# An attention and two feed-forward networks on one core: the token-side combinations of a seven-product block multiplication placed between the operations of neighbouring blocks

## The chip, the cores and the metric

The kernel runs on one core of a Trainium2 chip. The metric is the device time of one execution in microseconds, the median of several runs. A core has TensorE (PE in the profile), VectorE (DVE), ScalarE (ACT), GpSimd (POOL) and SyncE (SP), which here only issues DMAs. Each engine runs its own instructions in order and waits on semaphores.

## What is computed

```
attention: 2 batches x 8 heads, 768 tokens, head size 64; queries and keys meet only
           where the signs of six projections (proj) agree; softmax with eps 1e-9
x   = the attention's output, 1536 tokens x 512
y   = (h - tanh(h)) @ w_out,     h = x @ w_in        (w_in 512 x 2048)
out = sum over 4 experts e of  p[:, e] * (relu(y @ w1[e]) @ w2[e])     (w1[e] 512 x 1024)
      p = domain_probs / (their sum over e + 1e-9)
```

All is float32. To keep float32 accuracy with TensorE's faster rounded format, each operand is split in a rounded part (hi) and the rest (lo), and each product is made of three: lo*hi + hi*lo + hi*hi.

## The kernel before

**Attention.** Sixteen heads go in eight pairs (`pair(it)`, it = 0 to 7), each pair in twelve tiles t of 128 queries. For a tile PE scores it, VectorE takes the row's extreme (`clamp`), ACT the exponential (`take_exp`), PE turns it, ACT rounds what was turned (`round_turned`, pT_hi), VectorE makes the rest (`rest_turned`, pT_lo), and PE multiplies with the values (`weigh`). POOL prepares the queries and keys of later heads, adds eps to the sums (`add_eps`), adds the halves of a result (`x_add`) and scales it into acc (`x_scale`). After the last pair the engines finish the last head: VectorE inverts its sums (`invert`), adds (`last_sum`) and scales it (`last_scale`) itself; the inverse goes by DMA through DRAM into inv_rows (`spread_inverse` on SP).

**The two networks.** The hidden units come in groups of 256: 8 groups in the first network, 16 in the second. A pass i takes two groups and has four blocks r = 0 to 3: r // 2 is the half b of the tokens (768 each), r % 2 the group. I1 = 4: blocks (0,0) to (3,3) belong to the first network, (4,0) = (I1,0) and later to the second. A block's upward product is made by seven products instead of eight (`product`, L1393, six matmuls each): both the weights and x^T are cut in quadrants, and sums of quadrants are multiplied. So there are seven combinations, slots 0 to 6, on the weight's side (`up_sums` on POOL, `up_round` on ACT, `up_rest` on POOL) and seven on the token side, made once for each call c: c = 0 and 1 for the two token halves in the first network, c = 2 and 3 in the second. Slots 0, 1, 2 are plain quadrants of acc, slots 3 to 6 sums: `x_sum` for slots 3, 4, 6 on VectorE (L989, xq_raw) and for slot 5 on POOL (L521); `x_round` on ACT (L728, xq_hi); `x_rest` for slots 0, 1, 3, 4 on VectorE (L1001, xq_lo) and for 2, 5, 6 on POOL (L530). The xq_raw of slots 3 to 6 lies in the place of xq_lo, so that the sum is overwritten by the rest.

**A block's order.** PE (`place_block`, L1433): product 0 (P0), P1, one tile of the previous block's downward product (D0), P3, D1, P4, the product with x slot 2 (P6,2), tiles D2 to D4, P5, the rest of the tiles, and the product with x slot 6 (P(2,6)). A tile of the first network is 384 wide and there are eight, in the second 512 and six. ACT copies what P0, P3 and P4 left (`take_c1`, `take_c5`, `take_c2`, L795, L800, L805), VectorE adds the other products (`first`, `second_part`, `third`, L1107, L1112, L1117) and takes the down tiles (`down`). Between them the nonlinearity: ACT's tanh (L782), VectorE's subtraction (`hidden_sub`, L1128), ACT's rounding (L810) and POOL's rest (`hidden_rest`, L616) in the first network; ACT's relu (L858) and VectorE's rest (`positive_rest`, L1197) in the second. P4 waits for c1, P(6,2) for c5, P5 for c2, and P(2,6) for `third`'s h22. `down_round` (L736) and `down_rest` (L1006) split the downward weights in blocks r = 0 and 1.

**Where the splits of x stand.** c = 0 lies in pairs 5 and 6 and one operation of pair 7, among the tiles. The others stand in one piece: c = 1 partly after (0,0), the rest after (0,1); c = 2 (`split_x(2)`) after (3,3) and c = 3 after (4,0), on all three engines:

```python
                for r in range(4):
                    stage1(I1 - 1, r)
                split_x(2)
                stage2(I1, 0, 0, 0, after1=True)
                split_x(3)
```

The upward weights of group 1 are loaded after pair 7, summed on POOL in block (0,0), rounded on ACT and finished on POOL there; block (0,1) is the first to use them. wu_raw holds one group at a time.

## Time and profile before

| | us |
|---|---|
| median of three runs | 1057.4 (1056.42 to 1058.4) |
| profiled execution | 1058.94 |
| its span, first to last instruction | 1056.9 |
| PE busy | 1005.9 (95%) |
| VectorE busy | 690.8 (65%) |
| ACT busy | 467.1 (44%) |
| POOL busy | 454.9 (43%) |

The span is one execution's; times in the rows count from its start. Attention runs to about 254 us, the first network to about 520 us, the second to the end. Matmuls are pipelined and their ends are modelled, so PE's busy time shows where it waits but not how close it is to its peak. The granted clock (PEclk) is a share of 2.4 GHz; it has two levels, 1.2 and 2.4 GHz, so that a share between is a mixture in time.

### The profile page before, as it was taken

The page shows a single profiled execution, that of the slowest core. Times are in us where ns is not written, and L with a number is a line of the kernel's source. Part 1 is how long each engine was busy: PE and PEld are TensorE (multiplying, and loading weights), DVE is VectorE, ACT ScalarE, POOL GpSimd, SP SyncE. Part 2 cuts the span into 40 slices and gives each one's busy share as a digit, 9 for nine tenths or more (in the row PEclk, how much of TensorE's full clock was granted, in tenths as well). Part 3 has the DMA queues.
Part 4 walks back from the last instruction along what each step waited for, and adds up shares of the span by engine and source line. Part 5 has one row for each costly group of instructions (what it writes and reads, how often), then busy time and mean ns, then how long its engine had stood idle before and what let it go on. Part 6 is the DMA issues. An engine that isn't in the chain of part 4 may idle for free.

```text
span 1056.9 us, 16509 instructions
## 1 busy us (share of the span) xinstructions
PE 1005.9 (95%) x5438; PEld 926.9 (88%) x5438; DVE 690.8 (65%) x1124; ACT 467.1 (44%) x850; POOL 454.9 (43%) x436
## 2 busy tenths in 40 slices
PE   7999999898789999999696999999999999999998
PEld 5999998787789999999686999989889889989987
DVE  6888888896765556465677555555655565565554
ACT  4788777877434434443542232323223232233321
POOL 3687778876456355462753221313223041221200
PEclk9999999999889999999998999999999999999999
DMA  4445454442100101010010010100101001010003
GB/s 128 136 130 147 128 133 133 127 122 65 40 1 21 60 20 40 19 53 27 20 41 20 21 40 20 55 24 20 60 20 40 20 21 58 20 59 13 27 1 119
DMA packets 48324, 59.50 MB, mean 56 GB/s; under 512 B 4928, under 2 KB 31648, under 8 KB 48288
## 3 DMA queue, kind: packets, MB, share of 16 engines
q1 hardware_dynamic: 48128, 58.68, 19.3%
q10 hardware_dynamic: 160, 0.39, 0.1%
q8 instruction: 16, 0.26, 0.1%
q14 instruction: 20, 0.16, 0.1%
HBM read 44.07 MB, written 3.19 MB: 45 GB/s over the span
## 4 chain that ended last, share of the span: by engine, by line
PE 58%; issue 6%; POOL 5%; DVE 3%; ACT 1%; POOLq 0%; DVEq 0%; ACTq 0%
PE ps L1398 27%; PE ps L1421 25%; PE ps L1429 6%; POOL wu_lo L550 2%; POOL g_lo L616 2%; DVE xq_raw L989 1%; DVE xq_lo L1001 1%; POOL wu_raw L540 0%; POOL wu_raw L536 0%; DVE acc L1142 0%; POOL wu_raw L543 0%; POOL wu_raw L538 0%; ACT g_hi L810 0%; ACT wd_hi L736 0%; ACT g_hi L858 0%
## 5 line engine op out<-in xcount | busy, mean ns | idle before, releaser
L1398 PE MATMUL ps<-xq_hi,wu_lo 128*128 128x384 f32 x672 | 230.8, 343 | 31.9 <-DVE xq_lo L1001 15.9
L1398 PE MATMUL ps<-xq_hi,wu_hi 128*128 128x384 f32 x672 | 229.0, 341 | 0.0
L1398 PE MATMUL ps<-xq_lo,wu_hi 128*128 128x384 f32 x672 | 228.9, 341 | 0.0
L550 POOL TENSOR_TENSOR wu_lo<-wu_raw,wu_hi 128x768 fp32r<-128x768 f32 (+1 forms) x48 | 106.7, 2238 | 252.9 <-ACT wu_hi L732 252.8
L1159 DVE SCALAR_TENSOR_TENSOR acc<-ps,p_norm,acc 128x512 f32<-128x512 f32 x180 | 134.9, 749 | 102.5 <-PE ps L1421 99.1
L1398 PEld LDWEIGHTS ps<-xq_hi,wu_lo 128*128 128x128 f32 x672 | 127.9, 190 | 41.7 <-issue 19.8
L1421 PE MATMUL ps<-wd_lo,g_hi 128*128 128x512 f32 x384 | 151.2, 394 | 0.0
L1421 PE MATMUL ps<-wd_hi,g_hi 128*128 128x512 f32 x384 | 151.1, 393 | 0.0
L1421 PE MATMUL ps<-wd_hi,g_lo 128*128 128x512 f32 x384 | 150.9, 393 | 0.0
L858 ACT ACTIVATE g_hi<-hb 128x384 fp32r<-128x384 f32 x96 | 50.3, 524 | 187.7 <-DVE hb L1117 121.8
L1398 PEld LDWEIGHTS ps<-xq_lo,wu_hi 128*128 128x128 f32 x672 | 128.2, 191 | 5.4
L1398 PEld LDWEIGHTS ps<-xq_hi,wu_hi 128*128 128x128 f32 x672 | 128.1, 191 | 0.0
L616 POOL TENSOR_TENSOR g_lo<-hb,g_hi 128x384 fp32r<-128x384 f32 x64 | 65.8, 1028 | 128.3 <-ACT g_hi L810 128.3
L687 ACT ACTIVATE prob<-prob,neg_max 128x768 f32<-128x768 f32 x96 | 90.2, 940 | 39.0 <-DVE prob L948 39.0
L955 DVE TENSOR_TENSOR pT_lo<-ps,pT_hi 128x512 fp32r<-128x512 f32 x144 | 94.5, 683 | 13.1 <-ACT pT_hi L694 12.4
L948 DVE TENSOR_SCALAR_CACHE_REDUCE prob<-ps 128x768 f32<-128x768 f32 x96 | 90.9, 948 | 5.2 <-PE ps L1315 5.2
L1326 PE MATMUL ps<-ident,prob 128*128 128x128 f32 x576 | 84.6, 278 | 9.0 <-DVE pT_lo L955 8.7
L1421 PEld LDWEIGHTS ps<-wd_hi,g_hi 128*128 128x128 f32 x384 | 72.2, 188 | 16.9
L1429 PE MATMUL ps<-g_hi,wd_lo 128*128 128x384 f32 x256 | 86.9, 340 | 0.0
L1429 PE MATMUL ps<-g_hi,wd_hi 128*128 128x384 f32 x256 | 86.8, 339 | 0.0
L1429 PE MATMUL ps<-g_lo,wd_hi 128*128 128x384 f32 x256 | 86.7, 339 | 0.0
L1142 DVE TENSOR_TENSOR acc<-ps,acc 128x384 f32<-128x384 f32 x112 | 61.4, 554 | 36.4 <-PE ps L1429 36.0
(118 smaller groups left out, 1814.9 us busy)
## 6 DMA issues: line engine op xcount, KB each, us to landing
wu_raw<-in_w SPq DMA_DIRECT2D x64, 128.0 KB, 2.4
wd_raw<-in_w SPq DMA_DIRECT2D x16, 512.0 KB, 3.4
q_raw<-in_qT SPq DMA_DIRECT2D x32, 192.0 KB, 3.2
k_raw<-in_kT SPq DMA_DIRECT2D x30, 192.0 KB, 3.3
wu_raw<-in_w_in SPq DMA_DIRECT2D x32, 128.0 KB, 2.3
wd_raw<-in_w_out SPq DMA_DIRECT2D x8, 512.0 KB, 3.5
v_raw<-in_vP SPq DMA_DIRECT2D x16, 192.0 KB, 2.8
inv_rows<-inv_dram SPq DMA_DIRECT2D x16, 192.0 KB, 3.2
```

What stands on the lines that cost most here:

```text
L550: rest = pool.tensor_tensor(wu[par][1][:, slots, :, :], wu_raw[:, slots, :, :], wu[par][0][:, slots, :, :].bitcast(F32), ALU.subtract)
L616: pool.tensor_tensor(g_lo[par][:, f, l * HALF:(l + 1) * HALF], hb[:, h, :], g_hi[par][:, f, l * HALF:(l + 1) * HALF].bitcast(F32), ALU.sub ...
L687: act.activation(prob[t % 3][:], prob[t % 3][:], ACT.Exp, bias=neg_max[:, t:t + 1], scale=-1.0, accum_out=total[:, t:t + 1]).then_inc(exp_ ...
L858: act.activation(to, u_ps[r % 2] if n == 3 else source, ACT.Relu).then_inc(g_hi_ready, 1)
L948: dve.tensor_scalar(prob[t % 3][:], score_ps[slot][:, 0:S], MASKED, None, ALU.min, ALU.min, accum_out=neg_max[:, t:t + 1]).then_inc(clampe ...
L955: dve.tensor_tensor(pT_lo_flat[:, cols], turn_ps[m % 3], pT_hi_flat[:, cols].bitcast(F32), ALU.subtract).then_inc(pT_lo_ready, 1)
L1142: dve.tensor_tensor(part_of, d_ps[k % 4][:, 0:HALF], part_of, ALU.add).then_inc(down_taken, 1)
L1159: dve.scalar_tensor_tensor(out=part_of, in0=source, scalar=scale, in1=part_of, op0=ALU.mult, op1=ALU.add).then_inc(down_taken, 1)
L1326: mm = pe.transpose(turn_ps[m % 3][:, at * P:(at + 1) * P], prob[t % 3][:, k * P:(k + 1) * P], ident[:])
L1398: mm = pe.matmul(to, w[:, wslot, k, :], x[:, xslot, k, :], start=start and k + m == 0, stop=k == 1 and m == 2, skip_group_check=not start)
L1421: mm = pe.matmul(to, x[:, f, rows], y[:, f, :], start=f + m == 0, stop=f == FC - 1 and m == 2)
L1429: mm = pe.matmul(to, x[:, f, rows], y[:, f, cols], start=f + m == 0, stop=f == FC - 1 and m == 2)
```

## The change

- The token-side combinations of c = 1, 2 and 3 all move to VectorE: slot 5's sum and the rests of slots 2, 5, 6 leave POOL. `stage1` and `stage2` get `begin` and `end`: in a block with `begin` VectorE makes the sums 3 and 4 and the rests of slots 0, 1, 3, 2, and in the next one, with `end`, the sums 6 and 5 and the rests of 4, 5, 6. They stand singly between the block's own operations, except in (0,0), where five of the six stand together after hidden_sub 2. The blocks are (0,0)/(0,1) for c = 1, (3,3)/(4,0) for c = 2, (4,1)/(4,2) for c = 3. ACT's roundings stand in the same blocks: 0 and 1 before the block's first tanh, 3 after the first rounding, 4 and 2 before the third part; 5 and 6 in the next block ahead of its weight roundings and of take_c2.
- PE waits for each slot's rest by itself, in the order in which the products use them.
- c = 0: the seven sums and rests on VectorE are cut in halves of 384 columns, one to a tile: t = 0 to 5 and 8 to 11 of pair 5, t = 5, 7, 9, 11 of pair 6. ACT's order of rounding becomes 0, 1, 3, 4, 2, 5, 6; POOL's rests of slots 2, 5 and 6 move by some tiles.
- Group 0's weights are rounded and finished two to three tiles earlier in pair 7. Group 1's are loaded in the middle of pair 7, summed at t = 9, rounded by ACT at t = 11 and finished on POOL before and after `add_eps(HEADS - 1, 1)` and `x_add`.
- (0,0): the last head's three `weigh` parts stand after P1, after P3 and before the down tiles instead of together; `move_last(1)` follows take_c2; `last_sum(1)` and both `last_scale` follow second_part.
- g_hi, g_lo and v_st change places in SBUF, so that group 1's weights can be written before the attention is over.

```diff
-        HI_ORDER = (0, 3, 2, 5, 1, 4, 6)
+        HI_ORDER = (0, 1, 3, 4, 2, 5, 6)
+        REST_ORDER = (0, 1, 3, 2, 4, 5, 6)
...
+                        if isinstance(it, int) and it == PAIRS - 1 and b == 0:
+                            sp.wait_ge(wu_lo_ready, 1)
+                            load_up(sp, w_in[:, G:2 * G])
...
-                            if t == 3:
-                                x_rest(0, 6)
-                            if t == 6:
-                                up_rest(0, 0, 0)
-                            if t == 7:
-                                up_rest(0, 0, 1)
+                            if t == 2:
+                                x_rest(6)
+                            if t in (3, 4):
+                                up_rest(0, 0, t - 3)
+                            if t == 9:
+                                up_sums(1)
...
                 pair(PAIRS - 1, last=True)
+                up_rest(1, 1, 0)
                 add_eps(HEADS - 1, 1)
                 x_add(PAIRS - 1, 0)
+                up_rest(1, 1, 1)
...
-                        if last and t == 4:
+                        if last and t == 2:
                             up_round(0, 0)
                         if last and t == 7:
                             down_round(0, 0)
+                        if last and t == TILES - 1:
+                            act.wait_ge(clamped, HEADS * QT)
+                            up_round(1, 1)
...
+                    if begin is not None and not start:
+                        x_round(begin, 0)
+                        x_round(begin, 1)
                     act.wait_ge(h11_ready, count_of(i, r) + 1)
                     take_tanh(i, r, 0, hb[:, 0, :])
...
+                    if begin is not None and not start:
+                        x_round(begin, 3)
+                    if end is not None:
+                        x_round(end, 5)
+                        x_round(end, 6)
...
+                        if isinstance(it, int) and it == PAIRS - 3 and t < 6:
+                            x_sum(0, (3, 4, 6)[t // 2], slice(t % 2, t % 2 + 1))
+                        if isinstance(it, int) and it == PAIRS - 3 and t >= 8:
+                            x_rest(0, DVE_REST[t // 2 - 4], slice(t % 2, t % 2 + 1))
...
                     down(0)
+                    if end is not None:
+                        x_sum(end, 6)
+                        x_rest(end, 4)
+                    if begin is not None and not start:
+                        x_sum(begin, 3)
                     hidden_sub(i, r, 0)
+                    if end is not None:
+                        x_sum(end, 5)
+                    if begin is not None and not start:
+                        x_rest(begin, 0)
                     down(1)
                     second_part()
                     down(2)
+                    if begin is not None and not start:
+                        x_sum(begin, 4)
+                    if start:
+                        last_sum(1)
+                        last_scale(0)
+                        last_scale(1)
                     hidden_sub(i, r, 1)
+                    if end is not None:
+                        x_rest(end, 5)
                     down(3, 4)
+                    if begin is not None and not start:
+                        x_rest(begin, 1)
...
+                stage1(0, 0, begin=1)
+                stage1(0, 1, end=1)
...
+                stage1(I1 - 1, 3, begin=2)
+                stage2(I1, 0, 0, 0, after1=True, end=2)
+                stage2(I1, 1, 0, 0, begin=3)
+                stage2(I1, 2, 0, 0, end=3)
+                stage2(I1, 3, 0, 0)
```

## Rows read from the trace of the kernel before

**Rows 1.** The page's 40 slices: granted clock of TensorE in tenths.
```profile
PEclk9999999999889999999998999999999999999999
```
**Rows 2.** Windows: length, then busy us (instructions) of PE, PEld, DVE, ACT, POOL, clock.
```profile
128.14:156.92 28.78, 28.75 (x189) 26.36 (x188) 24.68 (x50) 22.89 (x48) 22.41 (x28) 1.00 0.51 137
156.92:190.81 33.89, 31.50 (x191) 28.15 (x190) 29.97 (x54) 25.06 (x52) 27.40 (x30) 0.95 0.44 119
190.81:223.79 32.98, 29.61 (x192) 26.89 (x191) 28.05 (x52) 25.75 (x51) 26.88 (x30) 1.00 0.54 139
...
253.77:269.07 15.30, 10.40 (x59) 9.42 (x57) 8.96 (x12) 8.46 (x15) 10.54 (x10) 0.95 0.16 56
269.07:287.19 18.12, 18.12 (x90) 18.12 (x91) 11.62 (x19) 7.21 (x13) 5.58 (x5) 0.86 0.20 59
287.19:313.30 26.11, 18.68 (x92) 18.39 (x92) 20.12 (x22) 9.24 (x16) 13.73 (x9) 0.80 0.00 0
504.25:519.98 15.73, 15.73 (x91) 15.58 (x90) 8.64 (x16) 7.74 (x13) 10.79 (x11) 1.00 0.04 11
519.98:547.92 27.94, 18.72 (x91) 17.67 (x91) 21.83 (x22) 11.21 (x16) 18.27 (x11) 0.82 0.05 14
547.92:574.91 26.99, 18.02 (x80) 15.42 (x79) 23.57 (x24) 9.63 (x15) 15.03 (x8) 0.81 0.17 57
574.91:590.53 15.62, 15.62 (x79) 14.08 (x79) 8.13 (x13) 3.54 (x7) 0.00 (x0) 1.00 0.01 2
```
**Rows 3.** Waits of PE: who waited for whom, us in total, times, longest.
```profile
PE ps L1398 <- DVE xq_lo L1001: 15.9, 3, 8.2
...
PE ps L1398 <- ACT hb L800: 6.5, 1, 6.5
```
**Rows 4.** The chain of work in (0,2): start us, us, what.
```profile
288.10 2.62 DVE xq_raw L989
```
**Rows 5.** Timeline of DVE: start us, us, instruction, [idle before <-releaser].
```profile
254.54 1.29 DVE L955 TENSOR_TENSOR pT_lo<-ps,pT_hi 128x512 fp32r<-128x512 f32 x2
...
511.81 0.56 DVE L1112 TENSOR_TENSOR hb<-ps,hb 128x384 f32<-128x384 f32 x1 [1.55 <-PE ps L1398]
...
542.18 2.11 DVE L1197 SCALAR_TENSOR_TENSOR g_lo<-hb,g_hi 128x384 fp32r<-128x384 f32 x1
...
545.15 1.21 DVE L1006 TENSOR_TENSOR wd_lo<-wd_raw,wd_hi 128x1024 fp32r<-128x1024 f32 x1
...
548.94 0.96 DVE L989 TENSOR_TENSOR xq_raw<-acc 128x768 f32<-128x768 f32 x1
...
559.84 2.87 DVE L1001 TENSOR_TENSOR xq_lo<-xq_raw,xq_hi 128x768 fp32r<-128x768 f32 x2
...
568.83 0.75 DVE L1155 TENSOR_SCALAR acc<-ps,p_norm 128x512 f32<-128x512 f32 x1 [1.26 <-PE ps L1421]
```
**Rows 6.** Timeline of POOL, columns as before.
```profile
252.35 0.20 POOL L488 TENSOR_TENSOR total_eps<-total,eps 128x6 f32<-128x6 f32 x1 [3.32 <-ACT prob L687]
...
288.09 1.80 POOL L521 TENSOR_TENSOR xq_raw<-acc 128x768 f32<-128x768 f32 x1 [0.96 <-DVE acc L1083]
...
511.38 1.85 POOL L550 TENSOR_TENSOR wu_lo<-wu_raw,wu_hi 128x768 fp32r<-128x768 f32 x1
...
515.48 2.41 POOL L550 TENSOR_TENSOR wu_lo<-wu_raw,wu_hi 128x1024 fp32r<-128x1024 f32 x1
```
**Rows 7.** Timeline of ACT, columns as before.
```profile
253.40 0.48 ACT L708 ACTIVATE pv_other<-ps 64x384 f32<-64x384 f32 x1 [0.65 <-PE ps L1345]
...
507.00 1.71 ACT L732 ACTIVATE wu_hi<-wu_raw 128x1792 fp32r<-128x1792 f32 x1 [0.58 <-POOL wu_raw L543]
...
510.77 0.49 ACT L805 ACTIVATE hb<-ps 128x384 f32<-128x384 f32 x1 [0.44 <-PE ps L1398]
...
518.77 0.83 ACT L728 ACTIVATE xq_hi<-acc 128x768 fp32r<-128x768 f32 x1
...
539.52 1.04 ACT L736 ACTIVATE wd_hi<-wd_raw 128x1024 fp32r<-128x1024 f32 x1
```

More of the change, by code:

```diff
@@ L636, in stage1 @@
                         up_sums(2 * i + 2)
-                def split_x(c):
-                    x_sum(c)
-                    for slot in POOL_REST:
-                        x_rest(c, slot)
                 def stage2(i, r, more=True):
@@ L1191, in stage1 @@
                     hidden_sub(i, r, 2)
+                    if begin is not None and start:
+                        x_sum(begin, 3)
+                        x_rest(begin, 0)
+                        x_sum(begin, 4)
+                        x_rest(begin, 1)
+                    if begin is not None:
+                        x_rest(begin, 3)
+                    if end is not None:
+                        x_rest(end, 6)
                     down(6, 7)
+                    if begin is not None:
+                        x_rest(begin, 2)
                 def positive_rest(i, r, n, f, l):
@@ L1220, in stage2 @@
                     down(0)
+                    if end is not None:
+                        x_sum(end, 6)
+                        x_rest(end, 4)
+                    if begin is not None:
+                        x_sum(begin, 3)
                     positive_rest(i, r, 0, 0, 0)
+                    if end is not None:
+                        x_sum(end, 5)
+                    if begin is not None:
+                        x_rest(begin, 0)
                     down(1)
```

252 lines of the change are left out of this document (127 added, 125 removed).

## The prediction

> **What bounds the kernel now.** I read the page's clock slices first, then the windows by stage, then PE's waits, then the instructions of the bad stretches in order of time. The clock slices [rows 1] say where to look: TensorE holds its upper level, 2.4 GHz, except around 170 us, 265 to 315 us and 530 to 580 us. The windows [rows 2] give the price. A steady pair of heads takes 28.8 us with PE busy throughout, but the pair in which group 0 of the token side is combined takes 33.9 and the next 33.0: 9.3 us over. A steady block takes 15.7 us in the first network and 15.6 in the second. Against that block (0,1) takes 18.1, (0,2) 26.1, (I1,0) 27.9 and (I1,1) 27.0: 2.4 + 10.4 + 12.2 + 11.4 = 36.4 us over. (0,0) takes 15.3 for 42 products' matmuls and 12 of the attention, 54 at 15.7/90 = 0.174 us, 9.5 with the small turn: 5.8 us over. So the change's territory holds 51 us above steady running; the rest runs at PE's pace and gives nothing.
>
> PE's waits [rows 3] name VectorE's xq_lo for 15.9 us in three waits, the longest 8.2, and ACT's copy of z for 6.5, which was itself queued behind the split. The granted clock of those windows is 0.80 to 0.86 [rows 2]: after each long wait PE runs at 1.2 GHz for some microseconds, which is part of the excess.
>
> **What one combination costs.** Alone, an x operation on VectorE takes 0.96 us, next to POOL's operations of the split 2.6, and the chain shows why: it lasts 2.62 where POOL's own operation of 1.80 began 0.01 earlier [rows 4 to 6]. The two take turns: a VectorE operation with two SBUF inputs waits for POOL's running one and then needs 2.62 - 1.80 = 0.8 to 0.9. Beside POOL's shorter sums each takes 1.43 [rows 5]. (POOL's in turn waits.) So I cost an x operation at 0.96 plus what is left of POOL's operation: 0 to 2.4.
>
> **Part 1, attention (group 0 of x).** The same sums and rests stay on VectorE, but as 14 halves of about 0.5 us (the 384-wide operation, 0.56 to its end [rows 5]) where seven whole ones stood; ten fall in pair 5, four in pair 6. In the windows VectorE's busy time rises by 5.3 us for four operations and by 3.4 for three, 1.24 each, so meeting POOL costs 0.28 a time [rows 2]. Halves: 0.78 each, 7.8 and 3.1 us. Before, almost none of it was absorbed (5.1 and 4.2 us of growth for 5.3 and 3.4, the rest being ACT's roundings, which stay). VectorE idles 4.1 us in a steady pair; placed one to a tile, I let the halves use 3.0 of it in pair 5 and 1.5 in pair 6: 7.8 + 0.8 - 3.0 + 3.1 + 0.8 - 1.5 = 8.0, against 9.3. Gain 1. Bounds: nothing absorbed, 12.5 (3 worse); all 4.1 and 3.1 absorbed, 5.3 (4 better). The skill has a rule here, in the Trainium skill's Perfetto Trace Analysis, "Optimizing Scalar/DVE Operations": breaking up instructions can help where VectorE isn't saturated but makes others idle, each with an overhead of some 60 ns; by it alone the halves would sit at the better bound.
>
> **Part 2, the end of attention.** Group 1's weights are loaded, summed and rounded earlier: SP's four DMAs move ahead of the last inverse's, POOL's four sums to t = 9, up_round(1, 1) to the last tile of ACT, and up_rest(1, 1) on POOL to either side of add_eps. This removes the wait for wu_lo before (0,1) (part of (0,0)'s 5.8). But the 1.71 us rounding [rows 7] now stands on ACT ahead of the last two pT_hi. Worse, POOL's first rest, 1.85 [rows 6], waits for that rounding and stands ahead of add_eps (before: done at 252.55 [rows 6]), which VectorE's reciprocal waits for, and behind this are queued last_sum(0) and the two last pT_lo. ACT reaches the rounding at 253.9 [rows 7]: 253.9 + 1.7 + 1.85 + 0.2 = 257.7 for add_eps, then 0.2 + 0.6 + 1.29 [rows 5] gives pT_lo at 259.8, where it was 255.8. PE has two products until 256.0, then waits 3.8 us and probably drops to 1.2 GHz. From here on I set down end times, with my own allowance of 0.1 to 0.2 us for each step from engine to engine. The weigh parts now alternate with products and hide ACT's copies: part 0 261.1 at 1.2 GHz, P3 263.0, part 1 264.3, P4 265.7, P(6,2) 266.8, part 2 267.5, P5 268.6. VectorE: second_part 267.5, last_sum(1) after ACT's move_last 268.8, both last_scale 270.0 (I take inv_rows as landed), hidden_sub(1) 270.6, third 271.1. P(2,6) runs to 272.3, where (0,1) started at 269.07.
>
> **Part 3, c = 1, in (0,0) and (0,1).** In (0,0) ACT's roundings 0 and 1, 0.83 each [rows 7], stand ahead of tanh 2, so hidden_sub(2) ends at 274.1. Then six x operations run on VectorE in a lump, 5 x 1.0 and one that meets POOL's hidden_rest, 1.8: 280.9, and only behind them (0,1)'s hidden_sub and first(). ACT's roundings 3, 4, 2 and tanh 3 bring c1 to 280.6. PE does two products, two down tiles (D0 waits for hidden_rest until 276.0) and P3 by 279.1, then waits for P4 till 280.7. VectorE: first() 282.0, down(0) 282.5, sum 6 and rest 4 284.5, hidden_sub 285.1, sum 5 286.1. ACT: roundings 5 and 6 287.9, down_round, 1.04, 289.0, take_c2, 0.49 [rows 7], 289.4. P5 starts at 289.5 where D4 ended at 287.5; down_rest, 1.21, and x_rest(5) delay third() by another 1.2. (0,2) starts at 296.2 instead of 287.19 but then runs at 15.7 and not 26.1: (0,3) starts at 312 instead of 313.3. Gain 1. Bounds: if the end of attention hides its lump (3.8 less at part 2), 5; if 1.2 GHz lasts through (0,0), 3 worse.
>
> **Part 4, c = 2, in (I1-1,3) and (I1,0).** In (I1-1,3) ACT's two roundings delay c5 by 0.6 us, VectorE (8.6 us busy in a steady block [rows 2]) takes six more operations, and two of them meet POOL's wu_lo rests of 1.85 and 2.41 [rows 6]; up_rest of the next group also comes later, behind hidden_rest 1. (I1,0) starts at 521.5, not 519.98. There the 8.2 us wait is gone, since slots 0 to 3 are ready. New: VectorE enters 1.5 late, first() 525.6, down(0) 526.1, x_sum(6) behind hidden_rest 527.8, rest 4 behind one of POOL's sums 529.3; PE wanted P4 at 526.8 and waits 2.6. Then positive_rest(0) 530.4, x_sum(5) 531.9; ACT: roundings 5 and 6 533.6, up_round, 1.71, 535.3, down_round 536.3, take_c2 536.8; VectorE: second_part and down(2) 537.9, positive_rest(1), held by up_rest (2.11 beside the same work before [rows 5]), 540.1, x_rest(5) 541.0. PE was ready for P5 at 534.7 and waits 6.3, then runs a product at 1.2 GHz. The block ends at 548 as before (547.92). Gain 0; bounds: POOL met half as often, 4 better; the sums loaded later, 3 worse.
>
> **Part 5, c = 3, in (I1,1) and (I1,2).** POOL is idle in both but for sums. In (I1,1) VectorE's load is three adds of 0.56, four rests of 0.56, six tiles of 0.75, down_rest 1.21 [rows 5] and 6 x 0.96: 15.4 us in 15.6. It fits; third() comes 0.5 late. (I1,1) takes 16.1, not 27.0. In (I1,2), P4 waits 0.7 for slot 4 and P5 1.9 for slot 5 (x_sum(5), two roundings, c2, second_part, down(2), rest, x_rest(5) in a row), P(2,6) 0.9: 19.1 instead of 15.6. Gain 10.9 - 3.5 = 7.4. Bounds: 5 (every x operation meets a sum once more) to 11 (none of the new waits).
>
> The xsum, xlo and PE's new slot-by-slot waits cost nothing beside this: a wait already met is not seen in the rows. The memory moves change no row.
>
> **Sum.** 1 + 1 + 0 + 7.4 = 9.4 us. The profiled execution took 1058.9 with a span of 1056.9, 1.5 above the median 1057.4. 1058.9 - 9.4 - 1.5 = 1048.0.
>
> **Rivals.** (a) The single operations mostly find POOL idle and the queue behind them short. For it: POOL is busy for 10.8 of 15.7 us in a steady block with rests, but none in (I1,2) [rows 2]. Parts 1 to 5 then give 4 + 5 + 4 + 9 = 22: 1035. Chance 0.13. (b) The wait only changes its name: PE waits for take_c2 and h22 in all four blocks as long as it waited for xq_lo. For it: that is what part 4 gives. Against: at c = 3 POOL is out of the way. Then part 5 gives 2 and the others 0: about 1056. Chance 0.08. (c) Slower: VectorE becomes the bound through turn-taking with POOL. There are 33 x operations after attention; a steady block leaves VectorE 7.1 us [rows 2], six blocks 43. At 0.96 they need 32 and fit; at 2.6 each 86, 43 over, plus the 3.8 at the end of attention: 47 against the 42.2 now over in these blocks, so 1062. It decides from about 2.4 us a piece. Against: 2.6 occurs only where POOL runs the split itself, which goes away. Chance 0.06. The Trainium skill speaks against this move in the same section of Perfetto Trace Analysis: with VectorE saturated some work may go to GPSIMD, though sharing a port may spoil that. By it this rival decides; VectorE at 8.6 of 15.7 us isn't saturated. (d) My forecast: 0.73.
>
> **How the numbers follow.** The range reaches from near rival (a), 1037, to rival (b), 1056: it leaves out most of (a) and all of (c). A measurement of this kernel can tell about 0.2%, 2.1 us: faster means below 1055.3. (a), (d) and a quarter of (b) lie there, less a little of (d): 0.86; same 0.08, slower 0.06.
>
> **What would show it.** Right: PE's waits name xq_lo for under 6 us, and ACT's c2 copy or VectorE's h22 for more than before; one wait of 3 to 4 us before the first weigh after the last scores; (0,3) starting near 312 and the second network's second block near 548 with the third near 564; POOL's x operations three instead of twelve; pairs 5 and 6 together near 65.5 us. Wrong: no wait at the end of attention, (I1,0) in under 20 us, or x operations on VectorE with a mean above 2 us.

## The result, and the profile after

The changed kernel takes 1051.1 us in the median (1050.9 to 1051.8), beside 1057.3 (1056.4 to 1058.4) for the kernel before: ratio 0.994, 95% interval 0.9925 to 0.9959. The forecast was 1048.0 in a range of 1037 to 1056, with a chance of 0.86 for faster. The gain is 6.2 us and not 9.4. The profiled execution took 1051.0 with a span of 1049.2, against 1056.9 before.

First the clock slices, as in [rows 1]. One slice of 40 shows a share below 0.9, where three did. A 9 stands for anything from 0.9 up, so that shorter stretches at the lower level, such as those of the windows below, don't show here.

```profile
PEclk9999999999999999999989999999999999999999
```

Then the windows of the changed kernel that answer to [rows 2]: length in us, then busy us (instructions) of PE, PEld, DVE, ACT, POOL, the granted clock, the DMA share and GB/s. They are a steady pair, pair 5, pair 6, pair 7 up to the first product of (0,0), the blocks (0,0), (0,1), (0,2), and from 505.55 on (I1-1,3), (I1,0), (I1,1), (I1,2).

```profile
127.46:156.12 28.66, 28.62 (x189) 26.29 (x188) 24.67 (x49) 22.87 (x48) 22.41 (x28) 1.00 0.51 137
156.12:194.35 38.23, 33.83 (x205) 29.90 (x204) 34.91 (x59) 25.67 (x52) 27.81 (x31) 0.96 0.41 111
194.35:227.72 33.37, 28.71 (x175) 25.64 (x172) 28.09 (x54) 24.84 (x49) 24.46 (x28) 0.95 0.49 127
227.72:258.87 31.15, 28.73 (x189) 25.86 (x187) 27.12 (x51) 26.05 (x50) 23.39 (x24) 1.00 0.32 86
258.87:276.30 17.43, 11.73 (x58) 10.91 (x57) 7.51 (x13) 7.84 (x14) 8.16 (x6) 0.90 0.24 73
276.30:298.70 22.40, 18.26 (x91) 17.01 (x91) 18.79 (x26) 11.21 (x20) 4.30 (x4) 0.92 0.04 11
298.70:314.50 15.80, 15.80 (x93) 15.80 (x92) 9.25 (x18) 5.55 (x12) 5.50 (x6) 1.00 0.05 19
505.55:522.10 16.55, 16.17 (x92) 15.53 (x91) 12.09 (x17) 10.04 (x16) 10.51 (x9) 1.00 0.00 0
522.10:547.80 25.70, 19.75 (x90) 18.69 (x91) 19.54 (x26) 8.47 (x13) 11.41 (x8) 0.87 0.22 62
547.80:563.90 16.10, 16.06 (x79) 14.05 (x79) 11.68 (x18) 8.26 (x13) 2.88 (x4) 1.00 0.02 5
563.90:582.85 18.95, 16.34 (x80) 13.85 (x79) 14.41 (x21) 5.01 (x9) 0.00 (x0) 1.00 0.07 25
```

Reading it stage by stage against [rows 2], and against the place where each step was forecast to end:

| stage | before | forecast | after | gain |
|---|---|---|---|---|
| pair 5 to the first product of (0,0) | 96.9 | 95.5 | 102.8 | -5.9 |
| of it pairs 5 and 6 | 66.9 | 65.5 | 71.6 | -4.7 |
| first product of (0,0) to that of (0,3) | 59.4 | 58.2 | 55.6 | 3.8 |
| (I1-1,3) and (I1,0) | 43.7 | 43.7 | 42.3 | 1.4 |
| (I1,1) and (I1,2) | 42.6 | 35.2 | 35.1 | 7.5 |

Pair 5 also begins 0.8 us earlier in the profiled execution (156.12 for 156.92), so attention as a whole costs 5.1. The sum, -5.1 + 3.8 + 1.4 + 7.5 = 7.6, is the 7.7 us between the spans. The loss in attention, where a gain of 1 was forecast, is the large miss, and two other stages gave more than forecast. Each number is one profiled execution's; how far such stages repeat is said at the head of the experiments.

PE's waits, as in [rows 3] (who waited for whom, us in total, times, longest), name the same releasers with other sizes:

```profile
PE ps L1379 <- DVE pT_lo L968: 9.3, 8, 1.6
PE ps L1451 <- DVE xq_lo L1017: 8.6, 5, 4.1
PE ps L1451 <- DVE hb L1134: 2.2, 1, 2.2
...
PE ps L1451 <- ACT hb L799: 1.9, 1, 1.9
PE ps L1348 <- DVE inverse L1029: 1.8, 1, 1.8
...
PE ps L1398 <- DVE pT_lo L968: 1.7, 1, 1.7
PE ps L1451 <- POOL wu_lo L549: 1.4, 3, 0.5
...
PE ps L1451 <- ACT hb L794: 1.1, 2, 0.8
```

xq_lo fell from 15.9 to 8.6, ACT's copy c5, the forecast's "copy of z" (`take_c5`, hb, L794), from 6.5 to 1.1 in two, and the two waits at the end of attention (1.8 for the inverse, 1.7 for pT_lo before the first weigh) are new. The halves themselves can be seen in VectorE's timeline of pair 5 (start us, us, instruction, idle before it):

```profile
160.50 0.57 DVE L1003 TENSOR_TENSOR xq_raw<-acc 128x384 f32<-128x384 f32 x1
...
164.23 1.82 DVE L1003 TENSOR_TENSOR xq_raw<-acc 128x384 f32<-128x384 f32 x1
...
173.23 2.10 DVE L1003 TENSOR_TENSOR xq_raw<-acc,xq_raw 128x384 f32<-128x384 f32 x1
...
192.31 2.12 DVE L1017 TENSOR_TENSOR xq_lo<-acc,xq_hi 128x384 fp32r<-128x384 f32 x1
```

and beside them POOL's, same columns:

```profile
163.79 1.84 POOL L521 TENSOR_TENSOR xq_raw<-acc 128x768 f32<-128x768 f32 x1
...
173.08 1.83 POOL L475 TENSOR_TENSOR k_st<-k_raw,k_st 64x768 fp32r<-64x768 f32 x1
...
192.16 1.85 POOL L475 TENSOR_TENSOR k_st<-k_raw,k_st 64x768 fp32r<-64x768 f32 x1
```

Each long half starts 0.15 to 0.44 us behind an operation of POOL and ends 0.42 behind its end: 163.79 + 1.84 = 165.63 and 164.23 + 1.82 = 166.05; 174.91 and 175.33; 194.01 and 194.43. A half alone takes 0.55. The 14 halves take 16.4 us, 1.17 each; the forecast had 0.78 each, 10.9. The seven whole operations before took 9.3, which is 0.36 each above their own 0.96.

### The profile page after: what moved, and what is told of

Read it like the earlier page. It is cut to its first block, busy times and chain, and to the rows that moved or that the text cites. A ratio compares the mean times of both kernels' runs of the same rounds, so it can differ in the third digit from the quotient of the medians.

```text
span 1049.2 us, 16514 instructions
## 1 busy us (share of the span) xinstructions
PE 1006.5 (96%) x5438; PEld 924.4 (88%) x5438; DVE 687.4 (66%) x1143; ACT 466.9 (44%) x850; POOL 424.5 (40%) x424
## 3 DMA queue, kind: packets, MB, share of 16 engines
q1 hardware_dynamic: 48128, 58.68, 19.5%
## 4 chain that ended last, share of the span: by engine, by line
PE 74%; DVE 9%; issue 8%; POOL 6%; ACT 2%; DMA 1%; POOLq 0%; SPq 0%; ACTq 0%; DVEq 0%
PE ps L1451 27%; PE ps L1474 24%; PE ps L1482 6%; PE ps L1368 5%; PE ps L1398 5%; PE ps L1379 4%; PE ps L1342 2%; POOL wu_lo L549 2%; POOL g_lo L617 2%; DVE xq_lo L1017 2%; DVE xq_raw L1003 2%; DVE pT_lo L968 1%; DVE prob L961 1%; ACT xq_hi L719 1%; POOL wu_raw L539 0%
## 5 line engine op out<-in xcount | busy, mean ns | idle before, releaser
L1451 PE MATMUL ps<-xq_hi,wu_lo 128*128 128x384 f32 x672 | 229.5, 342 | 15.9 <-DVE xq_lo L1017 8.6
L1379 PEld LDWEIGHTS ps<-ident,prob 128*128 128x128 f32 x576 | 67.9, 141 | 20.0 <-DVE pT_lo L968 14.4
```

The source lines that it names most:

```text
L1379: mm = pe.transpose(turn_ps[m % 3][:, at * P:(at + 1) * P], prob[t % 3][:, k * P:(k + 1) * P], ident[:])
L1451: mm = pe.matmul(to, w[:, wslot, k, :], x[:, xslot, k, :], start=start and k + m == 0, stop=k == 1 and m == 2, skip_group_check=not start)
```

## The experiments

All times are medians of 4 to 10 executions, to be held against 1051.1 for the changed kernel. They were taken on three chips, on which the kernel before had medians of 1058.0 (the first four experiments), 1056.8 (one input, c2 ahead, group 3 as before, the parts together) and 1057.0 (the last four), so a difference of 1 us or less says nothing. The second number given is the length of a stage in the trace, one execution each. Behind attention, stages with the same code repeat within 1.1 us: from the first product of (0,0) to that of (0,3) five kernels that are alike there (the changed one, whole operations, one input, group 3 before, group 3 in a lump) took 55.6, 56.5, 56.5, 56.7 and 55.8; (I1,0) took 25.5 to 26.7 in nine. Attention with halves repeats within 4 only, which the last section takes up.

**Whole operations at the new tiles.** The halves were merged, each pair at the tile of its second half.

```
-  it == PAIRS - 3 and t < 6:   x_sum(0, (3, 4, 6)[t // 2], <half t % 2>)
-  it == PAIRS - 3 and t >= 8:  x_rest(0, DVE_REST[t // 2 - 4], <half>)
-  it == PAIRS - 2 and t in (5, 7, 9, 11): x_rest(0, ..., <half>)
+  it == PAIRS - 3 and t in (1, 3, 5): x_sum(0, (3, 4, 6)[t // 2])
+  it == PAIRS - 3 and t in (9, 11):   x_rest(0, DVE_REST[t // 2 - 4])
+  it == PAIRS - 2 and t in (7, 11):   x_rest(0, DVE_REST[2 + t // 11])
```

> The changed kernel, with the 14 half operations of attention merged to the seven whole ones, each placed at the tile where its second half stood (1, 3, 5, 9, 11 of pair 5; 7, 11 of pair 6). Theory: what the halves cost too much is that each piece waits anew for the rest of POOL's running operation (halves took 1.15 us in the mean where 0.55 is their time alone, 15.0 us for 13 records; before, seven whole ones took 9.2). Whole ones should take about 1.35 each, 9.5 us in all against 16, and pairs 5 and 6 together 71.6 - 5 = 67 us: time 1046 to 1048. Rival 1: the loss comes from which tiles they stand at (five early ones in a row beside the bits step), so that pairs 5 and 6 stay at 71 us and the time at 1051. Rival 2: the loss comes from something else in the change (order of the roundings, the third network-side rest later), and neither the halves nor their tiles matter: 1051 too.

Measured: 1045.9 (1045.2 to 1046.5), 5.3 below the changed kernel. Pairs 5 and 6 in its windows:

```profile
155.72:188.62 32.90, 29.76 (x191) 26.70 (x190) 30.09 (x54) 25.19 (x52) 26.16 (x29) 1.00 0.45 122
188.62:221.02 32.40, 28.53 (x185) 25.90 (x184) 27.97 (x51) 25.21 (x50) 27.38 (x30) 1.00 0.53 136
```

65.3 us instead of 71.6, VectorE busy for 58.1 instead of 63.0, the clock at 1.00 in both where the changed kernel had 0.96 and 0.95. Its seven operations take 2.08, 0.99, 1.83, 0.99, 1.82, 1.74 and 1.72, 11.2 in all. Less 0.96 each that is 0.64 of waiting for POOL a piece; the halves' 1.17 less 0.55 is 0.62. The mean price of meeting POOL is the same for a piece of either size, and there were twice as many pieces. Rivals 1 and 2 (the tiles, the rest of the change) would have left 1051.

Not all of the 6.3 us is PE's waiting for longer pieces. The halves took 16.3 to 16.4 us in all in each of the seven profiles that have them, but the clock differed. Here are pair 5 of the kernel with late weights and pair 6 of the one with group 3 as before, both with halves and at 1.00:

```profile
156.52:193.48 36.96, 32.54 (x205) 28.57 (x204) 34.90 (x58) 25.68 (x52) 27.80 (x31) 1.00 0.43 114
194.98:226.72 31.74, 27.10 (x175) 24.16 (x173) 28.09 (x54) 24.85 (x49) 24.50 (x28) 1.00 0.52 133
```

Together that is 68.7 us, an estimate of what the halves take at the full clock. Halves against whole ones are so 3.4 us there, and 2.9 more are the stretches at 1.2 GHz in the changed kernel's profile.

**Attention's token side as before.** The old tiles on all three engines, whole operations, the old order of the roundings.

```
+  HI_FIRST = (0, 3, 2, 5, 1, 4, 6)                  # group 0 only
   DVE  +  PAIRS - 3: x_sum at t = 3, 6, 9, x_rest(0, 0) at 4;  PAIRS - 2: x_rest at 4, 7, 10
   POOL +  x_rest(2) at PAIRS - 3, t = 9;  x_rest(5) at PAIRS - 2, t = 3;  x_rest(6) at the last pair, t = 3
   POOL -  up_rest(0, 0, .) at t = 3, 4   +  at t = 6, 7;   ACT - up_round(0, 0) at t = 2   + at t = 4
```

> The changed kernel with everything that concerns group 0 of x and group 0's weights in attention as it was before: whole operations, the old tiles on all three engines, the old order of the roundings. Group 1's early weights and the token-side combinations of the three later groups stay changed. Theory: attention's loss of 5.1 us is wholly part 1's, so pairs 5 and 6 take 66.9 us as before and the time falls by 5 to 1046. Rival: half of it or more comes from the early loads, sums and rounding of group 1's weights or from the new memory layout; then the time is 1048.5 or more. Against the whole operations at the new tiles this run tells place from size.

Measured: 1048.0 (1047.5 to 1049.1), 3.1 below, not 5. Pair 5 to the first product of (0,0) takes 97.0 us, as before (96.9): so attention's loss is wholly this part's. At these tiles a piece pays 0.38 us for meeting POOL (9.4 us in all), and yet pairs 5 and 6 take 67.0, more than the 65.3 with 11.2 at the new tiles; the clock of pair 5 is 0.95 here. The price thus depends on the tile too, and VectorE's time alone doesn't set PE's. But from there to (0,3) it takes 58.5 us, 2.9 more than the changed kernel, since group 0's weights, split later, hold the one buffer wu_raw: POOL's sums of group 1 wait for the load, and all behind them comes later. The waits there (who for whom, us, times, longest):

```profile
DVE inverse L1030 <- POOL total_eps L495: 6.1, 1, 6.1
...
PE ps L1350 <- DVE inverse L1030: 3.7, 1, 3.7
...
POOL wu_raw L536 <- DMA wu_raw<-in_w_in: 3.9, 1, 3.9
```

The earlier split of group 0's weights is thus needed for the early load of group 1's. I had taken the two apart.

**Group 1's weights as late as before.**

```
   SP   -  load_up(w_in[:, G:2G]) in the last pair      +  behind spread_inverse
   POOL -  up_sums(1) at t = 9, up_rest(1, 1, .) after attention   +  in stage1(0, 0)
   ACT  -  up_round(1, 1) at the last tile              +  in stage1(0, 0), ahead of take_c2
```

> The changed kernel with group 1's up weights loaded, summed, rounded and split in block (0,0) as before, not in attention. Theory: the early weights remove the wait for wu_lo before (0,1) and cost the wait of 3.5 us for pT_lo before the weigh steps; undoing them brings the first back (about 3 to 5 us before (0,1), since the rests cannot be done before about 275) and removes the second, and the six x operations at the end of (0,0) now meet POOL's rests of the weights: time 1051 to 1055, (0,1) starting near 19 us after (0,0). Rival: the early weights brought nothing, since the wait of 3.5 us is as long as the one removed: 1051 or a little below.

Measured: 1054.4 (1051.5 to 1056.8), 3.3 slower. From the first product of (0,0) to that of (0,3) it takes 59.8 us instead of 55.6; PE waits 8.1 us for one ACT copy, queued behind the rounding that waits for the loads:

```profile
PE ps L1444 <- ACT hb L791: 10.0, 2, 8.1
```

That wait is for c2, where the 6.5 of [rows 3] was for c5; its kind is the same. The rival, that the early weights bring nothing, falls.

**EPS first on POOL.**

```
   pair(PAIRS - 1, last=True)
-  up_rest(1, 1, 0)
   add_eps(HEADS - 1, 1)
   x_add(PAIRS - 1, 0)
+  up_rest(1, 1, 0)
   up_rest(1, 1, 1)
```

> The changed kernel with one thing changed: on POOL, the last addition of EPS and the last sum of x stand ahead of the first weight rest and not behind it. Theory: the reciprocal waited 4.2 us for that addition, behind POOL's rest of 1.8 us and ACT's rounding of 1.7; with the addition first the reciprocal is done by 258 and pT_lo follows ACT's pT_hi (261.2), so the wait of 3.5 us before the first weigh step shrinks to about 1 and (0,0) takes 15 us instead of 17.4: time 1048.5 to 1049. Rival: the wait only moves on to the next late step (ACT's copy of o, the last scale of x, the six x operations), and the time stays within 0.5 us of 1051.

Measured: 1046.6 (1045.1 to 1050.2), 4.5 below. The wait for the inverse is gone and that for pT_lo is 1.33 where the two were 3.5; (0,0) to (0,3) takes 51.9 us instead of 55.6. In the first line the reciprocal has no idle time before it; in the second PE waits for pT_lo, now for the reason that ACT's rounding stands ahead of pT_hi:

```profile
260.96 0.18 DVE L1029 RECIPROCAL inverse<-total_eps 128x6 f32<-128x6 f32 x1
```
```profile
265.12 0.41 PE L1398 MATMUL ps<-pT_lo,v_st 128*128 128x384 f32 x1 [1.33 <-DVE pT_lo L968]
```

2.1 us of waiting less gave 3.7 us against the changed kernel's 55.6, and up to 4.8 against the longest profile with the same code there. The four executions run from 1045.1 at a mean clock of 0.995 to 1050.2 at 0.987, and the profiled one is the last of these, with an attention 2.1 us longer than the changed kernel's; so no trace places the rest of the median's 4.5.

**Halves with one input.** The kernel leaves out group 0's subtractions: its sums and rests are copies of one input, so that they have the same size, tile and number.

```
-  made = dve.tensor_tensor(x_raw[...ks...], one[:, ks, :], other[:, ks, :], ALU.subtract)
+  made = dve.tensor_copy(x_raw[...ks...], one[:, ks, :])          # c == 0
-  made = dve.tensor_tensor(x_lo[...ks...], raw[:, ks, :], x_hi[...], ALU.subtract)
+  made = dve.tensor_copy(x_lo[...ks...], raw[:, ks, :])           # c == 0
```

> The changed kernel with its 14 half operations at the same tiles and of the same size, each as a copy of one of its two SBUF inputs: the subtraction is left out for group 0 (its sums and rests are copies), nothing else. Theory: a half is long (1.15 us in the mean against 0.55 alone) only because an operation with two SBUF inputs on VectorE takes turns with POOL's. A copy with one input should never show a turn: all 14 at one duration near their shortest, below 0.6 us, pair 5 near 31 us instead of 38 and pair 6 near 30, the time 1042 to 1045. Rival: the halves are long because of the moment they stand at, or every access beside POOL is slowed alike; then copies scatter up to 2 us too and the time stays at 1049 or more.

Measured: 1043.3 (1042.5 to 1044.1), pairs 5 and 6 at 31.9 and 31.3 us: the time came out as the theory had it. Its stated sign did not. Ten of the 14 took 0.34 to 0.60, but four took 0.87 to 1.46, and these lines of VectorE show why:

```profile
164.16 1.46 DVE L1004 COPY xq_raw<-acc 128x384 f32<-128x384 f32 x1
...
167.62 0.34 DVE L1004 COPY xq_raw<-acc 128x384 f32<-128x384 f32 x1
...
220.68 1.25 DVE L1021 CAST xq_lo<-xq_raw 128x384 fp32r<-128x384 f32 x1
```

with POOL's beside them:

```profile
163.54 1.86 POOL L521 TENSOR_TENSOR xq_raw<-acc 128x768 f32<-128x768 f32 x1
...
219.86 1.85 POOL L475 TENSOR_TENSOR k_st<-k_raw,k_st 64x768 fp32r<-64x768 f32 x1
```

The first ends at 165.62, 0.22 behind POOL's 165.40; the third at 221.93, 0.22 behind 221.71; the one between ran with POOL idle. Nine of the 14, five of the short ones among them, end 0.21 to 0.22 behind an operation of POOL of 1.0 us or more; two ran with POOL idle. A copy of one SBUF input takes turns with POOL as well. It costs less (9.2 us for 14, against 16.4) because it needs only 0.2 once its turn comes, and meets POOL for a shorter time. So this run shows that attention's time follows the time of these pieces, and not that two inputs are the cause. The Trainium skill, in SBUF — State Buffer, "🔬 SBUF: two separate sides", has this wider form: copies in a mode with two ports are in the same exclusive lock as operations with two SBUF inputs. The trace agrees with the turns (0.21 to 0.22 us in each of the nine); in which mode the copies ran it doesn't show.

**c2 ahead.** In the blocks (0,1), (I1,0) and (I1,2) alone:

```
   ACT     x_round(end, 5)
+          take_c2(i, r, ...)
           x_round(end, 6)
           up_round(2 * i + 1, 1); down_round(2 * i, 0)     # where the block has them
-          take_c2(i, r, ...)
   DVE +   x_rest(end, 5)
           hidden_sub(i, r, 1)   /  positive_rest(i, r, 1, 0, 1)
-          x_rest(end, 5)
```

> The changed kernel with a new order inside the three blocks (0,1), (I1,0) and (I1,2): ACT's copy c2 stands directly behind the rounding of slot 5, ahead of that of slot 6 and of the weights' roundings, and VectorE's rest of slot 5 ahead of hidden_sub(1) or positive_rest(1). Theory: the three waits for P5 (1.9, 4.1 and 0.9 us) hang on that chain; up_round and down_round, 2.7 us, leave it in (I1,0), down_round in (0,1), 1.0, and positive_rest(1), 2.1: the wait of 4.1 falls to 1 or less and the 1.9 to 1; with the part at 1.2 GHz behind them 3 to 4 us less, 1047 to 1048. Rival: the weights' roundings that now come later hold POOL's rests and with them the next block's first product, or ACT's tanh(1); the waits change their name and the time stays at 1051 or rises to 1053.

Measured: 1048.1 (1047.7 to 1051.5), 3.0 below, as the theory had it. In the trace it is less clean: (0,0) to (0,3) takes 1.3 less ((0,1) alone 2.1), (I1,0) 24.0 instead of 25.7, (I1,2) 18.4 instead of 19.0, but (I1,1) 17.9 instead of 16.1, at a clock of 0.89, so some 1.7 in all, hardly more than the scatter of such stages. In (I1,0) the wait of 4.1 us for slot 5 went, and one of 3.3 for slot 6 took its place, behind down_rest, which lasted 2.5 us beside POOL's weight rests; so the rival was right by half there. (I1,1) begins right behind that wait. The profiled execution was the slowest of the four.

**Group 3 as before.** Its combinations alone, in one lump between (I1,0) and (I1,1), shared by VectorE and POOL.

```
-  stage2(I1, 1, begin=3); stage2(I1, 2, end=3)
   DVE  +  x_sum(3, 3), x_sum(3, 4), x_sum(3, 6); x_rest(3, slot) for slot in (0, 1, 3, 4)
   POOL +  x_sum (slot 5); x_rest for slot in (2, 5, 6)
   ACT  +  x_round(3, slot) for slot in (0, 3, 2, 5, 1, 4, 6)
```

> The changed kernel with the combinations for group 3 alone as before: in one lump between (I1,0) and (I1,1), shared by VectorE (three sums, four rests) and POOL (one sum, three rests), in the old order of roundings. Theory: part 5 of the forecast, 7.4 us, is this placement's worth; (I1,1) takes 27 us again and (I1,2) 15.7, the time rises to 1058.5. Rival: the lump's cost depends on the state in which PE comes to it, and since (I1,1) now begins with shorter queues behind (I1,0), less than half comes back: 1054 or less.

Measured: 1058.6 (1057.7 to 1061.0), 7.5 slower, and its (I1,1) and (I1,2):

```profile
548.09:575.10 27.01, 18.95 (x80) 16.21 (x79) 22.35 (x21) 9.36 (x15) 14.84 (x8) 0.81 0.05 19
575.10:590.71 15.61, 15.61 (x79) 14.06 (x79) 8.13 (x13) 3.54 (x7) 0.00 (x0) 1.00 0.01 3
```

27.0 and 15.6, which are the windows before [rows 2]. Part 5 of the forecast is confirmed on its own, 7.4 forecast and 7.5 measured.

**Group 3 in a lump, all on VectorE.** This parts who does it from where it stands.

```
-  stage2(I1, 1, 0, 0, begin=3); stage2(I1, 2, 0, 0, end=3)
+  for slot in (3, 4, 6, 5): x_sum(3, slot)
+  for slot in REST_ORDER:   x_rest(3, slot)
```

> The changed kernel with group 3's eleven combinations all on VectorE, as changed, but in one lump between (I1,0) and (I1,1), where the kernel before has them, and not singly. It parts the two things that the change does there at once: who does the work and where it stands. With both undone the time was 1058.6, 7.5 above 1051.1. Theory: both count. Eleven operations at 0.95 us hold VectorE for 10.5 us ahead of first() of (I1,1), where before two engines took turns for 11.4; PE has some 5 us of work before it needs that, waits for about 5 and runs slowly behind it, so (I1,1) takes 23, (I1,2) 15.7 again: 3.6 us slower than the changed kernel, 1054.5. Rival 1, only the engine counts (no turns with POOL): 1052 or less. Rival 2, only the place counts: 1058 or more.

Measured: 1056.4 (1055.0 to 1058.5), 5.2 slower.

```profile
549.57:573.62 24.05, 18.00 (x80) 15.51 (x80) 20.36 (x25) 9.20 (x15) 5.26 (x4) 0.86 0.07 21
573.62:589.23 15.61, 15.61 (x80) 14.06 (x79) 8.13 (x13) 3.54 (x7) 0.00 (x0) 1.00 0.01 2
```

(I1,1) takes 24.1 us where 23 were expected. In the sum of the two blocks, 42.6 with both undone, 39.7 with VectorE alone and 35.1 as changed, the engine is worth 3 us and the place 4.6 (by the medians 2.3 and 5.2). Both count, the place more.

**Group 1 as before.** Two combinations between (0,0) and (0,1), the rest behind (0,1), shared with POOL; the diff has the form of group 3's.

```
-  stage1(0, 0, begin=1); stage1(0, 1, end=1)
   DVE  +  x_sum(1, 3), x_rest(1, 0) behind (0,0);  x_sum(1, 4), x_sum(1, 6), x_rest(1, 1 / 3 / 4) behind (0,1)
   POOL +  x_sum (slot 5), x_rest for slot in (2, 5, 6), behind (0,1)
```

> The changed kernel with the combinations of group 1 of x alone as before: two of them between (0,0) and (0,1), the rest in a lump behind (0,1), shared by VectorE and POOL, in the old order of the roundings. The forecast gave this part 1 us; the trace of the changed kernel shows 3.8 from the first product of (0,0) to that of (0,3), together with the early weights. Theory: the new placement is worth 3 to 5 us, since the lump's 10.4 us over in (0,2) come back and (0,0) and (0,1) shorten by 4 to 6: 1054 to 1056. Rival, the forecast's size was right and the rest came from the weights: 1051.5 to 1053.

Measured: 1052.3 (1049.7 to 1052.9), 1.1 slower: the rival. In its trace (0,0) to (0,3) takes 58.0 us, 2.4 more than changed. Beside the run with late weights (59.8) and the kernel before with both undone (59.4), each of the two changes alone gives 1.4 and -0.4, and both together 3.8: with late weights ACT's queue is held until the load is there, wherever the roundings of x stand. The other kernels with the changed (0,0) and (0,1) took up to 56.7, so the 2.4 may be as little as 1.3. The size of the share that belongs to group 1 alone, 1.1 by the times or 1.3 to 2.4 by the traces, stays open.

**The parts together.** Whole operations, EPS first, c2 ahead, and ACT's rounding behind the last pT_hi:

```
-  if last and t == TILES - 1: act.wait_ge(clamped, HEADS * QT); up_round(1, 1)
   round_turned(HEADS - 1, QT - 1)
+  act.wait_ge(clamped, HEADS * QT)
+  up_round(1, 1)
```

> The changed kernel with what the runs so far favour, all at once: whole operations in attention at the tiles of the second halves (1045.9 alone), the last addition of EPS ahead of the weight rests on POOL (1046.6 alone, 2.5 to 3.7 us of it by its trace), ACT's rounding of group 1's weights behind the last two pT_hi and not ahead of them, and the order of c2 and slot 5 of the run beside it. Theory: the parts lie in different stages and add up: 5.3 + 3.5 + 1 + 3 = 13 us below 1051, 1038 to 1040. Rival: they share their gain (each removes the same half-clock stretch or the same queue), and it stays at 1043 or more.

Measured: 1038.0 (1036.6 to 1038.4), ratio to the kernel before 0.982 (0.980 to 0.984). The gains add up: 5.3 + 4.5 + 3.0 would be 12.8, it is 13.1.

**Other tiles.** On top of that, the seven whole operations at tiles where POOL waited for the score:

```
-  PAIRS - 3: t in (1, 3, 5), (9, 11);  PAIRS - 2: t in (7, 11)
+  PAIRS - 3: t in (2, 3, 8), 9;        PAIRS - 2: t in (2, 8, 9)
```

> The combined kernel (1038.0) with the seven whole operations of attention at other tiles: 2, 3, 8, 9 of pair 5 and 2, 8, 9 of pair 6, where in the traces POOL waits for the score and VectorE's operations ran at 0.54 to 0.99 us, in place of 1, 3, 5, 9, 11 and 7, 11, where three of seven took 1.7 to 2.1. Theory: what an operation costs there is its own 0.95 and what is left of POOL's; at the quiet tiles nearly all run at 0.95 to 1.1, VectorE saves some 3.5 us, and PE 2 of them: 1036. Rival: once whole, they are hidden or not as before whatever their length, and the time stays at 1038.

Measured: 1037.5 (1035.8 to 1038.9). The difference of 0.6 lies within the spread. In pair 5 the four operations took 0.95 to 1.24 and the pair 32.0 instead of 32.8; in pair 6 one took 1.98 and one 3.01, and the pair 35.0 instead of 32.5. Tiles at which POOL was idle in one profile aren't quiet in pair 6, where POOL has two rests of x of its own. Not a gain that can be told.

**Slot 6 ahead.** On top of the last one, in the same three blocks:

```
   DVE     x_rest(end, 5)
+          x_rest(end, 6)
           hidden_sub(i, r, 1)   /  positive_rest(i, r, 1, 0, 1)
-          down_rest(...)                                  # (0,1), (I1,0)
           third()
+          down_rest(...)
-          x_rest(end, 6)
```

> The combined kernel with the quiet tiles of the run beside it, and in the three blocks (0,1), (I1,0) and (I1,2) VectorE's rest of slot 6 directly behind that of slot 5, and down_rest of (0,1) and (I1,0) behind third(). In the combined kernel's trace the wait of 4.1 us in (I1,0) had not gone but moved from slot 5's product to slot 6's: its rest stood behind down_rest, which took 2.48 us beside POOL's weight rests. Theory: that wait falls below 1.5 us and PE stays at the upper clock in (I1,0), 3 to 4 us below the run beside it. Rival: P(2,6) then waits as long for third() or the next block for wd_lo, since VectorE has the same work: less than 1 us below.

Measured: 1030.5 (1029.5 to 1032.0), 6.9 below the run beside it and 26.5 below the kernel before; ratio 0.975 (0.973 to 0.976). (I1,0) in the run beside it, and then here:

```profile
511.99:536.05 24.06, 18.95 (x90) 18.18 (x91) 20.04 (x26) 8.38 (x13) 12.12 (x8) 0.88 0.22 65
```
```profile
511.02:529.76 18.74, 16.70 (x90) 15.63 (x91) 16.89 (x22) 8.37 (x13) 12.12 (x8) 1.00 0.10 28
```

PE's waits in the block fell from 5.1 to 2.0 us and the block by 5.3: the granted clock went from 0.88 to 1.00, and the mean clock of the whole execution is 1.00. The 6.9 is more than the 3 to 4 expected, since (I1,0) gave 5.3 and (I1,2) got 1.2 shorter too; what (0,1) gained, 0.9, (0,2) gave back but for 0.2.

## Why the prediction was right, and where it wasn't

**Part 1, attention: wrong, the largest term.** The step that failed is "Halves: 0.78 each", which took 0.28 for meeting POOL from the growth of VectorE's busy time with whole operations at their old tiles. Measured is 0.62 for a half and 0.64 for a whole one at the new tiles, so 16.4 us of VectorE where the sum had 10.9. A second term was not in the sum at all, the stretches at 1.2 GHz, though [rows 2] had pair 5 at 0.95 already: of the 6.1 us between 65.5 and 71.6, 2.9 are the clock's and 3.2 the longer halves' (68.7 at the full clock). That the absorption seems to have held was luck: 16.4 + 1.6 for ACT's roundings is 18.0, the two pairs took 14.0 more than steady ones, which looks like 4.0 absorbed for a forecast of 4.5, but at the full clock they took 11.1 more, so 6.9 were absorbed and the clock took 2.9 back. The 12.5 of the worse bound let nothing be absorbed but kept the 0.78, so the outcome lay outside it. Whole operations at the same tiles gave pairs 5 and 6 in 65.3 us, by chance what had been forecast for the halves, 65.5. What I should have seen stands in the forecast itself: "plus what is left of POOL's operation: 0 to 2.4" is paid for each piece, whatever its size. The Trainium skill's section on breaking up instructions (Perfetto Trace Analysis, "Optimizing Scalar/DVE Operations") names an overhead of some 60 ns a piece. For the fixed part the trace shows the same order, 2 x 0.55 for 0.96 alone, 0.14 more. What decided here, 0.6 us a piece of waiting for POOL, that section names only as a reason against moving work between the two engines, which share a read port.

**Part 2, the end of attention: the mechanism and the size held, its worth was not told apart.** Forecast 3.8 us of waiting before the first weigh, then 1.2 GHz; measured 1.8 + 1.7 = 3.5, and (0,0) at 17.4 us with the clock at 0.90, forecast 18.5. It came as two waits, the inverse's and pT_lo's, where one was written. POOL's order is the cause: turned round, (0,0) to (0,3) loses 3.7 us. The early weights themselves are worth 3.3 us, which the forecast did not state.

**Part 3, group 1: 3.8 us with part 2, forecast 1.** In (0,1), 22.4 for 23.9, and 21.6 to 22.3 in four other kernels alike there, each allowance I had made from engine to engine was a little long. In (0,0) the 17.4 for 18.5 is not such a gain: those four kernels took 18.5 to 18.9, in two of them with the same waits of 2.2, 1.8 and 1.7 us but at a clock of 0.81 and 0.82. The 3.8 is so 2.7 to 3.8. The chain was the right one, P5 waiting 1.9 us for ACT's copy (forecast 2.0). Of the 3.8, undoing group 1 alone takes back 1.1.

**Part 4, group 2: 1.4 us, forecast 0.** The order of events was as written: roundings, up_round, down_round, take_c2, second_part, positive_rest(1) held by POOL, x_rest(5). These lines of ACT and VectorE in (I1,0) show it:

```profile
531.91 1.58 ACT L719 ACTIVATE xq_hi<-xq_raw 128x768 fp32r<-128x768 f32 x2 [4.69 <-DVE xq_raw L1003]
533.39 1.68 ACT L723 ACTIVATE wu_hi<-wu_raw 128x1792 fp32r<-128x1792 f32 x1
...
534.98 1.04 ACT L727 ACTIVATE wd_hi<-wd_raw 128x1024 fp32r<-128x1024 f32 x1
...
535.92 0.47 ACT L799 ACTIVATE hb<-ps 128x384 f32<-128x384 f32 x1
...
537.64 2.07 DVE L1244 SCALAR_TENSOR_TENSOR g_lo<-hb,g_hi 128x384 fp32r<-128x384 f32 x1
539.63 0.95 DVE L1017 TENSOR_TENSOR xq_lo<-xq_raw,xq_hi 128x768 fp32r<-128x768 f32 x1
```

x_rest(5) ends at 540.6, forecast 541.0. But the waits were shorter, 1.85 instead of 2.6 for P4 and 4.10 instead of 6.3 for P5. Counted from the block's first product, x_rest(5) ended at 18.5 us instead of 19.5, and PE was there at 14.5 instead of 13.2, since behind the wait for P4 it ran 30 matmuls in 7.0 us at a clock of 0.76, where I had 5.3 (529.4 to 534.7):

```profile
529.61:536.62 7.01, 7.01 (x30) 6.69 (x30) 2.85 (x4) 4.49 (x5) 4.25 (x4) 0.76 0.00 0
```

The low clock behind the first wait thus hid a part of the second. The gain of 1.4 is 0.4 to 1.6 if one goes by the eight other kernels with the same code in these two blocks (42.1 to 43.2 us), and no run undid group 2 alone. The sign that I gave for this, "xq_lo under 6 us", failed with 8.6, because I had not added up my own waits (2.6 + 6.3 in this block alone).

**Part 5, group 3: right.** 16.1 and 19.0 us, forecast 16.1 and 19.1, its waits 0.77, 0.93 and 0.91 against 0.7, 1.9 and 0.9; undone, 7.5 us come back.

**The last step, from the profiled execution to the median: wrong by 1.6.** I took off 1.5 us because the profiled execution before lay that far above the median. The one after lay 0.15 below its own. The 13 runs of before beside the first experiments reach from 1056.4 at a mean clock of 0.983 to 1058.9 at 0.979, with a median of 1058.0, and the profiled one had 0.979; so the 1.5 was scatter and no property of the profile. The miss of 3.1 is thus 1.5 from the parts (6.1 too little in attention, 4.3 too much elsewhere, which is 1.8 in the spans and 1.5 in the times around them) and 1.6 from here.

**The signs.** Held: the wait of 3 to 4 us (in two parts), ACT's c2 copy (1.9 us for 1.2) and VectorE's h22 (2.2 for 1.9) waited for longer, the second network's second block at 547.8 and the third at 563.9 (548 and 564), POOL's x rests three instead of twelve (with the sum of group 0, four x operations). The two times held only because errors cancelled: attention came 5.1 later, the blocks of groups 1 and 2 were shorter by 5.2. Failed: xq_lo under 6 us (8.6), pairs 5 and 6 at 65.5 us (71.6), (0,3) at 312 (314.5). None of the signs of being wrong came: (I1,0) took 25.7 us, and the 33 x operations of VectorE behind attention took 1.08 us in the mean, where above 2 was the sign and about 2.4 what rival (c) needed. So in the networks the work that left POOL took most of the meetings with it. **The rivals:** (a), POOL mostly idle, 1035, and (c), VectorE as the bound, did not occur as wholes, but (c)'s mechanism, taking turns with POOL, is what hit attention, piece by piece and without VectorE being full. (b), the wait changes its name, is what (I1,0) shows, and what the run with c2 ahead showed once more with slot 6.

## What to carry to other kernels

Where an operation on one engine must wait for the running operation of another, count meetings and not microseconds: here cutting in two doubled the price, 8.7 us of waiting for 14 halves and 4.5 for seven whole ones. What a meeting costs is what is left of the other engine's operation. When work is spread between the steps of a block, list what each queue then holds ahead of the next thing that TensorE needs, and put the copies and rests that it needs first; moving such items (the addition of EPS, a rounding of weights, a copy, two rests) gave 15 us here, from 1045.9 to 1030.5, less than 1 of it from the quiet tiles, more than twice what the change itself did. After each such move look for the wait under its new name.

## What the runs showed of the hardware

- A copy on VectorE with a single SBUF input waits for POOL's running operation too: nine of 14 ended 0.21 to 0.22 us behind it, and took up to 1.46 us for 0.34.
- What a piece still needs once POOL's operation is over is its own time less some 0.13 us: 0.81 to 0.82 for a whole operation of 0.96 (128x768, two inputs), 0.40 to 0.42 for a half of 0.55, 0.22 for a copied half of 0.34.
- Attention with halves does not repeat, and the granted clock is what differs. From pair 5 to the first product of (0,0) the profiles took 101.0 us with the clock of pairs 5 and 6 at 0.96 and 1.00 (group 1 before, group 3 before), 101.2 at 1.00 and 0.95 (late weights), 102.8 and 103.1 at 0.96 and 0.95 (the changed kernel, group 3 in a lump), 104.7 and 104.8 at 0.91 and 0.90 (c2 ahead, EPS first). The halves met POOL alike in all seven, 16.3 to 16.4 us in total. With whole operations the five took 96.4, 96.4, 97.0, 97.2 and 97.5. It differs between executions of one kernel as well: the ten with late weights run from 1051.5 at a mean clock of 0.989 to 1056.8 at 0.982. What sends the clock down in one execution and not in the other was not tried. So a few us more in one of the single experiments may be this, and their stage lengths were given beside the times for it.
- The granted clock gives back more than the wait: 2.1 us of waiting less gave 3.7 to 4.8 us at the end of attention, and 3.1 less gave 5.3 in (I1,0), where the mean clock of the block rose from 0.88 to 1.00.
